# Experts' first product: weights stationary and results by columns, one tile at a time on TensorE

## The reference, cut to what matters

```
x is (2304, 512), w1 is (8, 512, 1024), w2 is (8, 1024, 512)
do_compute = x @ w_skip > 0
e_idx = argmax(x @ w_gate),  gate_w = its softmax probability
for e in range(8):
    h = maximum(x[mine] @ w1[e], 0)
    y[mine] = gate_w[mine] * (h @ w2[e])
out[do_compute] = x + y
```

## Time and profile before

| | |
|---|---|
| median of three runs | 802.39 us |
| the profiled execution: its own time | 800.32 us |
| its span, first to last instruction | 798.6 us |
| mean granted TensorE clock | 0.988 of full |
| TensorE busy | 762.0 us (95%) |
| VectorE busy | 523.0 us (65%) |
| ScalarE busy | 347.6 us (44%) |
| HBM moved, mean | 113 GB/s |

### The profile page before, as it was taken

The page is one execution under the profiler, slowest core; times in us unless marked ns, Lnnn a source line. Parts: engine busy times, 40 slices in busy tenths (PEclk is TensorE's granted clock), DMA queues, the critical chain, the costliest instruction groups (busy, mean ns, idle before and its releaser), DMA issues.

```text
span 798.6 us, 15577 instructions
## 1 busy us (share of the span) xinstructions
PE 762.0 (95%) x5170; PEld 642.8 (80%) x5171; DVE 523.0 (65%) x1331; ACT 347.6 (44%) x830; POOL 244.6 (31%) x240
## 2 busy tenths in 40 slices
PE   5999999797999999999999999999988999999995
PEld 3777777686899888888988988898866777887884
DVE  3888888743335984896697498536665897367342
ACT  3888888633322223222322322323442875346231
POOL 4888888843510210120020021000112122222211
PEclk9999999999999999999999999999998999999998
DMA  9566656442242122110210200411433798164000
GB/s 162 131 161 162 160 160 184 150 132 72 67 176 96 44 73 79 43 39 1 102 38 21 88 23 27 172 39 54 140 114 119 227 362 319 46 226 151 33 15 9
DMA packets 104966, 88.17 MB, mean 110 GB/s; under 512 B 66676, under 2 KB 82436, under 8 KB 104784
## 3 DMA queue, kind: packets, MB, share of 16 engines
q1 hardware_dynamic: 99488, 81.89, 33.9%
q0 software_dynamic: 3056, 5.00, 1.9%
q10 hardware_dynamic: 2368, 0.59, 0.4%
HBM read 72.26 MB, written 18.34 MB: 113 GB/s over the span
## 4 chain that ended last, share of the span: by engine, by line
PE 82%; ACT 5%; DVE 4%; issue 3%; SPq 3%; DMA 2%; DVEq 1%; POOL 0%; ACTq 0%; POOLq 0%
PE out_ps L1748 11%; PE h_ps L1748 11%; PE h_ps L1749 11%; PE out_ps L1750 11%; PE out_ps L1749 11%; PE h_ps L1750 11%; PE o_ps L696 5%; PE s_ps L680 3%; ACT prob L553 3%; PE t_ps L605 2%; SPq L86 2%; PE out_ps L1884 1%; PE s_ps L675 1%; ACT pt L537 1%; DMA attn_t<-attn_sb 1%
## 5 line engine op out<-in xcount | busy, mean ns | idle before, releaser
L1573 ACT ACTIVATE ex<-h_ps 128x384 f32<-128x384 f32 x96 | 47.3, 493 | 273.7 <-PE h_ps L1750 273.5
L1748 PE MATMUL h_ps<-xt_hi,wi_hi 128*128 128x384 f32 x384 | 132.1, 344 | 0.0
L1749 PE MATMUL h_ps<-xt_lo,wi_hi 128*128 128x384 f32 x384 | 130.1, 339 | 0.0
L1750 PE MATMUL h_ps<-xt_hi,wi_lo 128*128 128x384 f32 x384 | 130.0, 339 | 0.0
L1408 DVE TENSOR_SCALAR ex<-ex 128x384 f32<-128x384 f32 x96 | 36.6, 381 | 136.2 <-ACT ex L1573 134.8
L1748 PE MATMUL out_ps<-wo_hi,gt 128*128 128x512 f32 x288 | 115.3, 400 | 4.0 <-DVE gt L1401 4.0
L1750 PE MATMUL out_ps<-wo_hi,gt 128*128 128x512 f32 x288 | 114.6, 398 | 0.0
L1749 PE MATMUL out_ps<-wo_lo,gt 128*128 128x512 f32 x288 | 114.0, 396 | 0.0
L553 ACT ACTIVATE prob<-s_ps,negmax 128x128 f32<-128x128 f32 (+2 forms) x144 | 77.8, 556 | 14.7 <-DVE negmax L413 13.8
L1290 DVE CUSTOM_DVE_ANT_0 x2t<-x,w_raw 128x512 bf16<-128x512 f32 x108 | 82.7, 806 | 0.4
L1186 POOL TENSOR_TENSOR xt_lo<-x_raw,xt_hi 128x384 fp32r<-128x384 f32 x20 | 28.3, 1413 | 166.6 <-ACT xt_hi L1590 166.4
(11 more groups left out here) (180 smaller groups left out, 1589.5 us busy)
## 6 DMA issues: line engine op xcount, KB each, us to landing
w_raw<-in_moe_w_dram SPq DMA_DIRECT2D x56, 512.0 KB, 5.3
raw_qk<-in_q_dram SPq DMA_DIRECT2D x32, 144.0 KB, 3.0
attn_t<-attn_sb SPq DMA_DIRECT2D x16, 288.0 KB, 2.1
x_raw<-attn_t SPq DMA_DIRECT2D x24, 192.0 KB, 2.4
out_dram<-x SPq DMA_DIRECT2D x18, 256.0 KB, 2.1
x_rows<-x SPq DMA_DIRECT2D x18, 256.0 KB, 2.7
v<-in_v_dram SPq DMA_DIRECT2D x32, 128.0 KB, 2.5
wi_raw<-in_moe_w_in_dram SPq DMA_DIRECT2D x16, 256.0 KB, 2.8
```

What stands on the lines that cost most here:

```text
L1573: act.activation(ex[:, f % 2], h_ps[:, f % 2, 0:NB], ACT.Exp).then_inc(ex_done, 1)
L1748: pe.matmul(dst, stat[0], mov[0], start=start, stop=False, skip_group_check=True)
L1749: pe.matmul(dst, stat[0], mov[1], start=False, stop=False, skip_group_check=True)
L1750: return pe.matmul(dst, stat[1], mov[0], start=False, stop=stop, skip_group_check=True)
```

## The change

`hidden` now takes a 128x128 block of **w1 as the stationary operand** and the **token block (128 columns) as the moving one**. Each result block is hidden columns by tokens, which is what `output` needs, and four of them fill one bank. So the transposes of h, the copy `h_sb`, and `relu` go; ScalarE's `ht_high` applies Relu from the product's bank while rounding, and VectorE's `ht_low` takes max(h, 0) minus the high part from the same bank. On TensorE each tile is done by itself: both halves of `hidden`, `turn_x` of the next tile, the whole `output`. The reads of the tile count (`ask`) come behind a tile instead of in it, and the waits for w2 stand at each piece inside `output`. Nothing changes in attention, in the feed-forward stage, in the loads, gathers and scatters.

```diff
             def ht_low(t, j):
                 dve.wait_ge(ht_hi_done, HALVES * t + j + 1)
-                dve.tensor_tensor(ht[1][:, j * KC:(j + 1) * KC, :],
-                                  ht_ps[:, j].rearrange("p (k t) -> p k t", k=KC),
-                                  ht[0][:, j * KC:(j + 1) * KC, :].bitcast(F32),
-                                  ALU.subtract).then_inc(ht_lo_done, 1)
+                dve.scalar_tensor_tensor(ht[1][:, j * KC:(j + 1) * KC, :],
+                                         hm_ps[:, j].rearrange("p (k t) -> p k t", k=KC), 0.0,
+                                         ht[0][:, j * KC:(j + 1) * KC, :].bitcast(F32),
+                                         ALU.max, ALU.subtract).then_inc(ht_lo_done, 1)
...
             def other(e, i, t):
-                if not is_zero(e):
-                    ht_low(t - 1, 1)
                 row(t)
                 ht_low(t, 0)
+                ht_low(t, 1)
                 xt_low(t + 1)
...
-            def relu(t, j):
-                wait(act, ht_done, HALVES * t)
+            def ht_high(t, j):
                 act.wait_ge(hm_done, HALVES * t + j + 1)
-                act.activation(h[:, j * BANK:(j + 1) * BANK], hm_ps[:, j], ACT.Relu)\
-                   .then_inc(relu_done, 1)
-
-            def ht_high(t, j):
-                act.wait_ge(ht_done, HALVES * t + j + 1)
-                if not is_zero(t):
-                    act.wait_ge(ym_done, t)
                 act.activation(ht[0][:, j * KC:(j + 1) * KC, :],
-                               ht_ps[:, j].rearrange("p (k t) -> p k t", k=KC),
-                               ACT.Copy).then_inc(ht_hi_done, 1)
+                               hm_ps[:, j].rearrange("p (k t) -> p k t", k=KC), ACT.Relu).then_inc(ht_hi_done, 1)
...
                     for j in range(PIECES):
                         w2_high(e, i, j)
-                    relu(t, 0)
+                    ht_high(t, 0)
                     next_w1(act, e, i, w1_high, [0, 1])
-                    ht_high(t, 0)
-                    next_w1(act, e, i, w1_high, [2])
-                    relu(t, 1)
+                    ht_high(t, 1)
                     xt_high(t + 1)
-                    next_w1(act, e, i, w1_high, [3])
+                    next_w1(act, e, i, w1_high, [2, 3])
...
                     if not is_zero(t):
-                        pe.wait_ge(relu_done, HALVES * (t - 1) + j + 1)
+                        pe.wait_ge(ht_lo_done, HALVES * (t - 1) + j + 1)
                 for k in ks:
                     if e is not None:
                         pe.wait_ge(w1_lo, PIECES * e + k + 1)
-                    last = mm3(hm_ps[:, j], [x[:, k, :] for x in mxt],
-                               [w[:, k, j * BANK:(j + 1) * BANK] for w in w1_sb[i]],
-                               k == 0, k == KC - 1)
+                    for f in range(j * KC, (j + 1) * KC):
+                        last = mm3(hm_ps[:, j, (f - j * KC) * P:(f - j * KC + 1) * P],
+                                   [w[:, k, f * P:(f + 1) * P] for w in w1_sb[i]], [x[:, k, :] for x in mxt],
+                                   k == 0 and f == j * KC, k == KC - 1)
...
-            def tile(e, i, t, before, ask=lambda: None):
-
-                if before is not None:
-                    outputs(before, t - 1)
+            def tile(e, i, t):
+
                 hidden(e, i, t, 0)
-                if before is not None:
-                    output(before, t - 1, range(EARLY, FCE))
-                ask()
-                hidden(None, i, t, 1, range(TURN_K))
-                turn_h(t, 0)
-                hidden(None, i, t, 1, range(TURN_K, KC))
+                hidden(None, i, t, 1)
                 turn_x(t + 1)
+                output(e, i, t)
```

More of the change, by code:

```diff
@@ L780, in experts @@
     HALVES = FE // BANK
-    TURN_K = 2
-    EARLY = KC
     HALF = FC // 2
@@ L869, in experts @@
         sb("gap1", [P, 2 * KC * NB - 2 * FE], F32)
-        h = sb("h_sb", [P, FE], F32)
-        sb("gap2", [P, 4 * NB - FE], F32)
+        sb("gap2", [P, 4 * NB], F32)
         assert nc.sbuf_base == end
@@ L920, in experts @@
         rk_ps = ctx.enter_context(nc.psum_tensor("rk_ps", [P, BANK], F32))
-        xt_ps, hm_ps, ht_ps, y_ps = tr_ps, h_ps, out_ps[:, 0:HALVES], out_ps[:, HALVES]
+        xt_ps, hm_ps, y_ps = tr_ps, h_ps, out_ps[:, HALVES]
         const_done = sem("f_const_done")
@@ L1510, in first @@
                 else:
-                    if not is_one(e):
-                        ht_low(t - 1, 1)
                     for j in range(PIECES):
@@ L1515, in first @@
                     row(t)
-                    next_w1(dve, e, i, w1_low, [0])
                     ht_low(t, 0)
-                    next_w1(dve, e, i, w1_low, [1])
+                    next_w1(dve, e, i, w1_low, [0, 1])
+                    ht_low(t, 1)
                     xt_low(t + 1)
@@ L1523, in other @@
             def other(e, i, t):
-                if not is_zero(e):
-                    ht_low(t - 1, 1)
                 row(t)
                 ht_low(t, 0)
+                ht_low(t, 1)
                 xt_low(t + 1)
-                if is_zero(e):
-                    ht_low(t, 1)
             finish_attention = attend["vector"](dve)
@@ L1563, in _ @@
             total = all_tiles(dve)
-            ht_low(total - 1, 1)
             final(total - 1)
@@ L1708, in first @@
                     if not is_one(e):
-                        ht_high(t - 1, 1)
                         act.wait_ge(ym_done, t - 1)
@@ L1736, in _ @@
             soften(LAST, 1)
-            relu(0, 0)
+            ht_high(0, 0)
             soften(LAST, 2)
-            relu(0, 1)
+            ht_high(0, 1)
             over_experts(act, first, other)
-            total = all_tiles(act)
-            ht_high(total - 1, 1)
         @block.tensor
@@ L1865, in hidden, with output @@
                 if ks[-1] == KC - 1:
                     last.then_inc(hm_done, 1)
[L1868 to L1872, removed]
+            def output(e, i, t):
+                pe.wait_ge(final_done, t + 1)
+                for f in range(FCE):
                     if f % KC == 0:
                         pe.wait_ge(ht_lo_done, HALVES * t + f // KC + 1)
+                    if e is not None and f % (FCE // PIECES) == 0:
+                        pe.wait_ge(w2_lo, PIECES * e + f // (FCE // PIECES) + 1)
@@ L1875, in output @@
                     last = mm3(y_ps, [x[:, f, :] for x in ht], [w[:, f, :] for w in w2_sb[i]],
                                f == 0, f == FCE - 1)
[L1877 to L1892, removed]
-            def tile(e, i, t, before, ask=lambda: None):
-                if before is not None:
-                    outputs(before, t - 1)
-                hidden(e, i, t, 0)
-                if before is not None:
-                    output(before, t - 1, range(EARLY, FCE))
-                ask()
-                hidden(None, i, t, 1, range(TURN_K))
-                turn_h(t, 0)
-                hidden(None, i, t, 1, range(TURN_K, KC))
+                last.then_inc(ym_done, 1)
@@ L1905, in tile @@
+            def tile(e, i, t):
+                hidden(e, i, t, 0)
+                hidden(None, i, t, 1)
                 turn_x(t + 1)
+                output(e, i, t)
             def first(e, i, t, ask):
                 if is_zero(e):
-                    turn_h(0, 0)
-                    turn_h(0, 1)
-                    output(0, 0, range(FCE))
+                    output(0, 0, 0)
                     turn_x(1)
                     pe.wait_ge(route, ROUTED)
-                    ask()
                 else:
-                    pe.wait_ge(w2_lo, PIECES * e)
@@ L1917, in first @@
-                    tile(e, i, t, None if is_one(e) else 1 - i, ask)
+                    tile(e, i, t)
+                ask()
             def other(e, i, t):
[L1920 to L1926, removed]
+                tile(None, i, t)
             def first_hidden(f):
@@ L1955, in _ @@
             over_experts(pe, first, other)
[L1956 to L1959, removed]
 _INS = ['q', 'k', 'v', 'moe_w_in', 'moe_w_out', 'moe2_w_skip', 'moe2_w_gate', 'moe2_w1', 'moe2_w2']
```

8 lines of the change are left out of this document (removed).

## The result

The changed kernel took 869.67 us (median of 4 runs, 868.86 to 870.85), the one before in the same session 801.68 us (800.59 to 802.54): ratio 1.085, interval 1.0829 to 1.0871. The profiled execution took 868.86 us against 800.32 us, its span is 867.2 against 798.6 us: +68.6 us where +63.2 was forecast. The page's first part answers to the earlier trace rows.

A forecast was written before the change was run, and what follows sets the result against it. TensorE's program was taken to bound the experts: 13 periods +54.7, tile 1 +4.7, tile 0 +5.1, tail -1.3, in all +63.2 us on 800.32. With the runs' median 2.1 us higher, the forecast was 865 us, range 845 to 905.

The forecast's parts named there:

- What bounds the stage: Steady part of the experts: TensorE's program sets the period, 12.73 us a tile before, 16.94 us after.
- The price of a load, 0.111 us: First product: 96 matmuls each wait for a load of 0.111 us, 10.7 instead of 5.60 us, +5.1 a tile.
- rivals two to four: First-product matmul distance: series 0.17 us, about 950, 5%; four passes 0.218, about 1019, 5%; loads hidden 0.058, about 789, 2%.
- Order and cover: Tiles done serially: `ht`, x and w2 pieces are ready in time; first half's `ht` needs 3.7 us under 5.3.
- Tile 0's first product on the path: Tile 0, ahead of the count and routing: its longer first product delays everything later by 5.1 us, nothing hidden.
- Small waits: Each steady tile on TensorE: 0.2 us of small waits kept in the period, as before.
- Tile 1 pays that again, about as much.: Tile 1 after TensorE's idle time: the loss at the 1.2 GHz clock stays about as large as before.
- the term for tile 1: Tile 1, ahead of the 13 periods: 10.7 instead of 5.60 us, one group of transposes less, +4.7 us.
- granted clock 1.00 from 617 us on: Sign expected in the trace after: TensorE at full clock from 617 us on.
- rival 1: First products: clock falls to 1.2 GHz, distance 0.22 us, +224 us, about 1026 us; 7%.
- behind the last `turn_x`: End of the last tile: 5.80 us to the last matmul's start instead of 7.09, -1.3 us.

The follow-up runs named there:

- E1: Kernel before, each first-product matmul cut into four of 128 columns (96 loads a tile), x still stationary: 886.01 us, ratio 1.1106.
- E2: Kernel before, each first-product matmul cut into two of 256 columns (48 loads a tile): 801.57 us, ratio 1.0023.
- E4: Changed kernel with 256 instead of 128 moving columns in the first product, still 96 loads, results not the reference's: 868.88 us, ratio 1.0869.
- E7: Changed kernel with one load of w1's high block serving both halves of x, 64 loads a tile, plus a ScalarE copy and VectorE add: 825.07 us, ratio 1.0309.
- E3: Kernel before with only the changed one's order, each tile finished by itself, 512 columns and transposes kept: 805.66 us, ratio 1.0068.
- E6: Changed kernel plus 7 matmuls of 512 columns, results unread, between `turn_x(1)` and tile 1's first product: 859.71 us, ratio 1.0725.
- E10: Changed kernel with both fillings of unread 512-column matmuls, 16 ahead of tile 0's output and 7 ahead of tile 1's first product: 867.66 us, ratio 1.0802.
- E9: Changed kernel plus 16 matmuls of only 8 columns, results unread, ahead of tile 0's output: 883.37 us, ratio 1.1016.
- E5: Changed kernel plus 16 matmuls of 512 columns, results unread, ahead of tile 0's output: 882.15 us, ratio 1.1034.

## Why the prediction was right, and where it was wrong

- **What bounds the stage**: right. The steady part has no hole in 211.5 us, so the period is TensorE's program: 10.66 us, `turn_x` 0.38 us, and the output 5.69 us, 16.74 against 16.94 forecast.
- **The price of a load, 0.111 us**: right, and it is the step that carried the result. E1, E2 and E4 show that it is loads that are paid, whatever streams with them up to 256 columns; E7 that it scales with their number. The Trainium skill, "TensorE: Matmul & The Clock Gate", section "Back-to-back issue gap", gives some 81 ns for a stream of loads and matmuls at 128 columns. The trace does not agree: for float32r it is 0.111 us, and the measurement decides. Of the rivals two to four (in series, four passes, quick loads) nothing is left.
- **Order and cover**: right. `ht` is never waited for, while E3 and E7 show that the cover is not large: with the old turning, or one copy more, waits of up to 1.5 us are there.
- **Tile 0's first product on the path**: right, 5.0 us of 5.1 arrive at every later mark.
- **Small waits**: the 0.2 us a tile that I kept did not come. 13 x 0.2 = 2.6 us too much.
- **The mis-sized step: "Tile 1 pays that again, about as much."** By the term for tile 1, +4.7 us, its first product was charged 96 x 0.111 with the clock's loss as before, 1.6 us (7.67 less 5.60 and 0.44). It lost 8.1 us by itself (18.82 instead of 10.7), and the period behind it another 1.6. The step took a loss measured on 512 columns, which had the clock back within 3.5 us of their start (the row at 612.72 us lasts 0.39 us again, after 0.63), and gave it unchanged to a stream of 128 columns. That stream started tile 1 at the full clock, lost it 1.9 us later and did not get it back by itself, for 17 us. E6 takes the idle time ahead of tile 1 away and gets the 8 us back; E4, with twice the columns, had the clock back after 3.5 us. The sign "granted clock 1.00 from 617 us on" failed up to 636.4 us and held from there on; rival 1 came true in one tile of fourteen.
- The two sizes partly cancel: +6.4 in tile 1, +1.6 in the first period, -2.6 for the waits, -0.1 in tile 0 and +0.1 behind the last `turn_x` make the 5.4 us between +63.2 and +68.6.

That the total fits so well is in part luck: the two errors of the clock, 8.0 us together, stand against 2.6 us of waits that did not come.

Not settled: when a stream of 128 columns loses the clock (behind one hole of E10 and not behind the other, in E9 without a hole, never in the changed kernel's steady part), and which address a slow branch goes to.

## What to carry to other kernels

Cutting a product into narrower pieces is free until the streamed columns no longer hide the load: here that is between 256 columns (0.116 to 0.120 us) and 128 (0.111 us for half the work), so count loads, not columns, and put the operand that leaves the wide side moving. The stream bound by loads held the full clock in the steady part, where it alternates with 512 columns, but lost it in tile 1 and did not regain it until wide matmuls came; see what stands behind each idle stretch of TensorE, and put a few wide matmuls into the stretch if a narrow product follows (E6). Look at an edited loop's branches in the trace for ones of several microseconds before its cost is put down to what it computes.

## What the runs showed that I had not expected

- **A clock that does not rise.** In the changed kernel 16 us without a gap at 0.50 (76 matmuls of 128 columns), 18 us in E5, and in E9 14.6 us that no idle time preceded; yet 1.00 for 211.5 us with the same product in 64% of each period. The Trainium skill ("TensorE: Matmul & The Clock Gate", "What's actually happening") says that the engine's activity releases the clock; this stretch, busy throughout and still at 0.50, does not agree with it if busy time is taken for activity.
- **Slow branches.** The kernel before has none over 0.3 us among the experts; 16 instructions more in the changed one make two of 3.4 to 3.9 us. Of eight in E1, E5, E9 and E10 three hide behind queued matmuls and five leave TensorE idle for 1.3 to 2.9 us; in E5 that cost 2.1 us and, through the clock, 10 more.
- **Spread.** The kernel before ran between 795.2 and 805.2 us over these sessions, so a gain of 1 us in a stage is read from the trace and hardly from the time.
